# The second expert layer works in expert order, and half of its rows are fetched and transposed while the first layer ends

## The reference

```python
def _moe_ref(x, ...):                      # first layer: one expert for each token
    e_idx = np.argmax(logits, axis=1)
    for e in range(E):                     # E = 8, F = 1024
        mask = e_idx == e
        h = np.maximum(x[mask] @ w1[e], 0.0)
        out[mask] = gate_w[mask, None] * (h @ w2[e])

def _moe2_ref(x, w_gate, w1, w2):          # second layer: every expert for every token
    P = np.exp(x @ w_gate - max)
    for _ in range(8):                     # rows, then columns are scaled
        P /= P.sum(1, keepdims=True) + 1e-09
        P /= P.sum(0, keepdims=True) + 1e-09
        P *= N / E
    for e in range(E):
        out += P[:, e:e + 1] * (np.maximum(x @ w1[e], 0.0) @ w2[e])
```

## Time and profile before

| | us |
|---|---|
| median of 3 runs | 1403.03 (1402.81 to 1403.81) |
| profiled execution, its own time | 1405.03 |
| its span | 1403.0 |
| mean granted TensorE clock | 0.994 |
| TensorE busy | 1371.9 (98%) |
| VectorE / ScalarE / GpSimd busy | 705.2 / 450.6 / 416.4 |

### The profile page before, as it was taken

How to read it: one execution, slowest core, us unless ns; L and a number is a source line. 1 busy time by engine, 2 the same in 40 slices (tenths; PEclk the granted TensorE clock), 3 DMA queues, 4 the chain that set the end, 5 groups by cost and what they waited for, 6 DMA issues and landing times.

```text
span 1403.0 us, 21674 instructions
## 1 busy us (share of the span) xinstructions
PE 1371.9 (98%) x7515; PEld 1221.7 (87%) x7516; DVE 705.2 (50%) x1290; ACT 450.6 (32%) x867; POOL 416.4 (30%) x615
## 2 busy tenths in 40 slices
PE   8999989999799999999999999999999999999999
PEld 7999678888688888999988889999888999988888
DVE  8886672141464644445454444455444445544444
ACT  6887432232243422223131222313122222322221
POOL 4111022222430523415052332505143241605330
PEclk9999999999999999999999999999999999999999
DMA  6440372121301011101110010011101011110001
GB/s 131 107 105 32 129 245 72 42 75 38 136 31 31 30 30 31 31 31 30 45 45 30 30 30 30 30 45 45 30 30 30 30 30 37 43 39 30 30 32 58
DMA packets 95647, 73.85 MB, mean 53 GB/s; under 512 B 43344, under 2 KB 76144, under 8 KB 95600
## 3 DMA queue, kind: packets, MB, share of 16 engines
q1 hardware_dynamic: 92560, 65.34, 15.5%
q0 software_dynamic: 2672, 7.88, 1.7%
q10 hardware_dynamic: 368, 0.02, 0.0%
HBM read 62.74 MB, written 10.49 MB: 52 GB/s over the span
## 4 chain that ended last, share of the span: by engine, by line
PE 92%; DVE 4%; ACT 1%; issue 1%; POOL 1%; DMA 1%; POOLq 0%; SPq 0%; DVEq 0%; ACTq 0%
PE ps L2025 37%; PE ps L2000 33%; PE ps L1886 5%; PE ps L1864 5%; PE ps L1684 3%; PE ps L1618 1%; PE ps L1644 1%; PE ps L1873 1%; PE ps L1630 1%; PE ps L1678 1%; PE ps L1798 1%; PE ps L1603 1%; PE ps L1693 1%; PE ps L1933 1%; PE ps L1844 0%
## 5 line engine op out<-in xcount | busy, mean ns | idle before, releaser
L2000 PE MATMUL ps<-x_hi,w_hi 128*128 128x384 f32 x896 | 301.7, 337 | 4.7 <-DVE x_lo L1447 3.8
L1529 DVE SCALAR_TENSOR_TENSOR acc<-ps,mix,acc 128x512 f32<-128x512 f32 x180 | 135.1, 751 | 329.2 <-PE ps L2025 329.2
L2000 PE MATMUL ps<-x_hi,w_lo 128*128 128x384 f32 x896 | 300.5, 335 | 0.0
L2000 PE MATMUL ps<-x_lo,w_hi 128*128 128x384 f32 x896 | 300.3, 335 | 0.0
L2025 PE MATMUL ps<-w_hi,h_hi 128*128 128x512 f32 x768 | 300.0, 391 | 0.0
L2025 PE MATMUL ps<-w_hi,h_lo 128*128 128x512 f32 x768 | 299.7, 390 | 0.0
L2025 PE MATMUL ps<-w_lo,h_hi 128*128 128x512 f32 x768 | 299.4, 390 | 0.0
L739 POOL TENSOR_TENSOR w_lo<-w_raw,w_hi 128x256 fp32r<-128x256 f32 x224 | 159.0, 745 | 89.5 <-ACT w_hi L934 89.5
L2000 PEld LDWEIGHTS ps<-x_hi,w_hi 128*128 128x128 f32 x896 | 168.9, 188 | 7.6 <-DVE x_lo L1447 4.2
L2025 PEld LDWEIGHTS ps<-w_hi,h_hi 128*128 128x128 f32 x768 | 144.1, 188 | 32.9 <-DVE h_lo L1489 5.0
L2025 PEld LDWEIGHTS ps<-w_hi,h_lo 128*128 128x128 f32 x768 | 144.1, 188 | 30.6
(11 more groups left out here) (280 smaller groups left out, 1781.4 us busy)
## 6 DMA issues: line engine op xcount, KB each, us to landing
w_raw<-in_moe_w_dram SPq DMA_DIRECT2D x64, 256.0 KB, 3.0
w_raw<-in_moe_w_dram SPq DMA_DIRECT2D x16, 1024.0 KB, 5.3
stage<-in_moe_w_dram SPq DMA_DIRECT2D x8, 1024.0 KB, 6.4
first_raw<-in_moe_w_dram SPq DMA_DIRECT2D x4, 1024.0 KB, 8.1
q_raw<-in_q_dram SPq DMA_DIRECT2D x12, 256.0 KB, 3.4
k_raw<-in_k_dram SPq DMA_DIRECT2D x12, 256.0 KB, 4.3
v_all<-in_v_dram SPq DMA_DIRECT2D x12, 256.0 KB, 4.4
x_rows_dram<-x_rows SPq DMA_DIRECT2D x12, 256.0 KB, 4.0
```

What stands on the lines that cost most here:

```text
L1529: dve.scalar_tensor_tensor(out=acc[:, m, :], in0=ps[:, 4 + t % 3, :], scalar=mix_flat[:, bass.ds(e + m * (E + 1), 1)], in1=acc[:, m, :], o ...
L2000: last = pe.matmul(ps[:, bank, 0:CT], w_part[:, j, w, ks], x_part[:, x, k, cols], start=(opens and k == 0 and n == 0), stop=(k == 1 and n ...
```

## The change

**Order.** Results of the first layer stay in order by expert. Instead of scattering a block to its tokens, GpSimd writes it as 128 contiguous rows, starting at `row[b]` (`store_y`); where a block isn't full, the next store covers its tail, since stores are in order. VectorE works out the table `row` before the first layer's loop (7 small operations). The second layer then takes the rows in this order; at the very end the output tiles go to their tokens' rows by a scatter from GpSimd instead of a plain store from SyncE. The token numbers in expert order come from `token_places` (8 small VectorE operations), 12 scatters of 4 bytes per partition to DRAM on GpSimd behind `split_half(0, 1)`, and 12 small loads on SyncE at the end of expert 6.

**Early half.** As soon as the blocks that hold rows 0 to 767 are stored (here 8 of 14), SyncE loads these 6 tiles. They are combined between the last two rests of the first layer, and their seven operands are transposed one operand at a time (6 transposes for an operand): two before the last product's wait, one just before that product, one after it, three between the first products of `up(0, 0, 0)`. The pairs are now (i, i+3) and (i+6, i+9). The first w1 sums and rests move in front of the last stores on GpSimd. w2 is loaded when the last product2 is done, and its first rounding moves to `up(0, 0, 1)`, because w2_hi and w2_lo share memory with the early rows.

```diff
 # SyncE
             load_w1(0, 0)
             load_w1(0, 1)
+            half_done = sp.value_load(tab[0:1, TAB_H:TAB_H + 1], ...)     # blocks - 3
+            half_done = sp.snap(half_done >> 1, ...)
+            for c in range(2):
+                sp.wait_ge(y_buffer_free[c], half_done * 16)
+            for i in range(3):
+                for m in (i, i + 3):
+                    sp.dma_start(y_early[:, m, :], yd[:, m, :]).then_inc(y_loaded[i], 16)
...
+            sp.wait_ge(block_done, last_pair * 2 + 2)
+            load_w2(0, 0)
             sp.wait_ge(y_stored, 1)
-            for i in range(TILES // 2):
-                for m in (i, i + TILES // 2):
-                    sp.dma_start(y_rows[:, m, :], yd[:, m, :]).then_inc(y_loaded[m], 16)
-            load_w2(0, 0)
+            for i in range(3):
+                for m in (i + 6, i + 9):
+                    sp.dma_start(acc[:, m, :], yd[:, m, :]).then_inc(y_loaded[i + 3], 16)
 # GpSimd
-            for c in range(2):
-                scatter_y(last_pair, c, last_pair * 4 + (c + 2))
...
+            sums_w1(0, 0)
+            sums_w1(0, 1)
+            lows_w1(0, 0)
+            store_y(last_pair, 0)
+            lows_w1(0, 1)
+            store_y(last_pair, 1)
...
             hold(6).then_inc(y_stored, 1)
-            split_half(0, 0)
+            split_w2(0, 0)
...
             split_half(0, 1)
+            pool.wait_ge(places_ready, 1)
+            for m in range(TILES):
+                pool.indirect_dma_start(out=tokens_dram, out_offset=...token_place[:, m:m + 1]...,
+                                        in_=token_id[:, m:m + 1], ...).then_inc(tokens_placed, 16)
...
+                    pool.wait_ge(out_bank_free, 24 * (E - 1) + u * 6 + t + 1)
+                    pool.indirect_dma_start(out=out, out_offset=...row_token[:, m:m + 1]..., in_=acc[:, m, :], ...)
 # ScalarE
+            act.wait_ge(xr_loaded[0], last_pair * 16 + 32)
+            act.wait_ge(xr_loaded[1], last_pair * 16 + 16)
             w1_round(0, 0)
-            for i in range(3):
-                x2_round(i)
+            hT_round(last_pair, 1)
             w1_round(0, 1)
-            up_evacuate(0, 0, 0)
+            act.wait_ge(block_done, last_pair * 2 + 2)
+            for n in range(4):
+                early_round(n)
+            up_evacuate(0, 0, 0, after_p1=next_early, hook=lambda: early_round(6))
...
-                w2_now = u % 2 == 0 and j == 0
+                w2_now = u % 2 == 0 and j == (1 if begin and u == 0 else 0)
 # VectorE
+            hT_rest(last_pair, 0)
+            split_next(last_pair, 0)
             for i in range(3):
                 x2_combine(i)
-            for i in range(3):
-                x2_rest(i)
+            token_places()
+            y_evacuate(last_pair, 0)
+            hT_rest(last_pair, 1)
+            y_evacuate(last_pair, 1)
+            for n in range(4):
+                early_rest(n)
+            up_finish(0, 0, 0, after_u2=lambda: early_rest(4), after_u3=lambda: early_rest(5),
+                      after_c11=lambda: early_rest(6))
             x2_combine(3)
-            up_finish(0, 0, 0)
+            dve.wait_ge(y_stored, 1)
             up_finish(0, 0, 1)
 # TensorE
             transpose_h(last_pair * 2 + 2)
-            keep_busy(14, 0)
-            product2(1, last_pair * 2 + 1, last_pair * 2 + 2)
-            keep_busy(90, 0)
-            for i in range(3):
-                transpose_y(i)
-            up(0, 0, 0)
+            pe.wait_ge(x2_combined, 3)
+            transpose_early(0)
+            transpose_early(1)
+            keep_busy(4, 5)
+            pe.wait_ge(hT_split, last_pair * 2 + 2)
+            transpose_early(2)
+            product2(1, last_pair * 2 + 1, last_pair * 2 + 2)
+            pe.wait_ge(y_copied, last_pair * 2 + 2)
+            transpose_early(3)
+            up(0, 0, 0, behind={"P1": transpose_early_4, "P7": transpose_early_5, "P2": transpose_early_6})
```

More of the change, by code:

```diff
@@ L127, in attention_moe_moe @@
         idx_x = take("idx_x", [PART, 2], i32)
-        idx_y = take("idx_y", [PART, 2], i32)
+        token_id = take("token_id", [PART, TILES], i32)
+        place_f = take("place_f", [PART, TILES])
+        token_place = take("token_place", [PART, TILES], i32)
+        row_token = take("row_token", [PART, TILES], i32)
+        row_f = take("row_f", [PART, 24])
+        row = take("row", [PART, 24], i32)
         used = take("used", [PART, 1])
@@ L330, in attention_moe_moe @@
         table_ready = sem("table_ready")
+        rows_ready = sem("rows_ready")
+        places_ready = sem("places_ready")
+        tokens_placed = sem("tokens_placed")
+        row_tokens_loaded = sem("row_tokens_loaded")
         shifted = sem("shifted")
@@ L421, in tile_of @@
         def tile_of(u, t):
-            return (t // 3) * (TILES // 2) + (u % 2) * 3 + t % 3
+            return (u % 2) * (TILES // 2) + t
         def head_of(half, l):
@@ L749, in split_half, with store_y @@
             def split_half(e, hu):
-                split_w1(e, 2 * hu)
-                split_w1(e, 2 * hu + 1)
+                for p in (2 * hu, 2 * hu + 1):
+                    sums_w1(e, p)
+                    lows_w1(e, p)
                 split_w2(e, hu)
-            split_half(0, 0)
+            def store_y(i, c):
+                pool.wait_ge(y_copied, i * 2 + (c + 1))
+                pool.wait_ge(y_buffer_free[1 - c], i * 16 + (16 + 16 * c))
+                at_row = pool.value_load(row[0:1, bass.ds(i * 2 + c, 1)], min_val=0, max_val=N)
+                pool.dma_start(y_rows_dram[bass.ds(at_row, PART), :], y_blk[:, c, :]).then_inc(y_buffer_free[c], 16)
+            pool.wait_ge(rows_ready, 1)
+            with pool.Fori(0, PAIRS - 1) as i:
+                with pool.If(i < last_pair):
+                    for c in range(2):
+                        pool.wait_ge(xT_done, i * 2 + (c + 2))
+                        gather_x(i * 2 + (c + 3), 1 - c, i * 2 + (c + 2))
+                        store_y(i, c)
+            sums_w1(0, 0)
[4 more added lines that the diff above has]
+            store_y(last_pair, 1)
+            pool.wait_ge(y_buffer_free[0], pairs * 16 + 16)
+            pool.wait_ge(y_buffer_free[1], pairs * 16 + 16)
+            hold(6).then_inc(y_stored, 1)
+            split_w2(0, 0)
             pool.wait_ge(local_max, 1)
@@ L1975, in up @@
                 cols = slice((u % 2) * CT, (u % 2 + 1) * CT)
-                if begin and u < 2 and j == 0:
-                    pe.wait_ge(x2_split, 3 * u + 3)
+                if begin and u == 1 and j == 0:
+                    pe.wait_ge(x2_split, OPS + 3)
                 if u % 2 == 0:
                     pe.wait_ge(w1_split, e * 4 + (2 * (u // 2) + j + 1))
-                for name, bank, w, x in PRODUCTS:
+                for n, (name, bank, w, x) in enumerate(PRODUCTS):
+                    if first:
+                        pe.wait_ge(x2_split, n + 1)
                     if name == "P1" and not first:
@@ L1998, in up @@
                         ks = slice(k * PART, (k + 1) * PART)
-                        for n, (w_part, x_part) in enumerate(((w1_hi, x2_hi), (w1_hi, x2_lo), (w1_lo, x2_hi))):
+                        for h, (w_part, x_part) in enumerate(((w1_hi, x2_hi), (w1_hi, x2_lo), (w1_lo, x2_hi))):
                             last = pe.matmul(ps[:, bank, 0:CT], w_part[:, j, w, ks], x_part[:, x, k, cols],
-                                             start=(opens and k == 0 and n == 0), stop=(k == 1 and n == 2),
+                                             start=(opens and k == 0 and h == 0), stop=(k == 1 and h == 2),
                                              skip_group_check=True)
@@ L2031, in down @@
                             step()
-            for i in range(3):
-                transpose_y(i)
-            up(0, 0, 0)
+            transpose_h(last_pair * 2 + 1)
+            product1(1, last_pair * 2 + 1, last_pair * 2 + 2)
+            product2(0, last_pair * 2, last_pair * 2 + 1)
+            transpose_h(last_pair * 2 + 2)
+            pe.wait_ge(x2_combined, 3)
[8 more added lines that the diff above has]
+            up(0, 0, 0, behind={"P1": transpose_early_4, "P7": transpose_early_5, "P2": transpose_early_6})
             up(0, 0, 1)
```

254 lines of the change are left out of this document (147 added, 107 removed).

## The result

The changed kernel takes 1397.19 us, median of 7 runs (1395.80 to 1399.25), against 1403.03 us for the kernel before in the same job (7 runs, 1402.79 to 1404.72). The ratio is 0.9959, 95% interval 0.9947 to 0.9970: 5.8 us faster. Forecast were 1389.6 us, with a range of 1384 to 1397: the median lies 0.2 us above the range. The direction was right; less than half of the gain of 13.4 us came.

A forecast was written before the change was run, and what follows sets the result against it. TensorE, busy 98% of the span, was taken as the bound; down(0, 0) 16.7 us earlier, less 2.1 for one clock fall, with 1.2 added for the last store, gave -13.4 from 1403.03: 1389.6 us, range 1384 to 1397.

The forecast's parts named there:

- the last store: Kernel's end: a GpSimd scatter instead of a plain store adds 1.2 us (0.8 to 4.8).
- sign of a span end: Sign of being right: span ends 3.2 us or so after the last accumulation.
- Product2: First layer's last product: ends 3.1 us later than 360.83; its start 2 to 4 us after 355.09 was a sign.
- The combining: Twelve VectorE operations before the last product: 9.8 us beside GpSimd's work, bounds 5.0 and 11.4 us.
- The w2 wait: Before down(0, 0): TensorE waits about 3.2 us for GpSimd's w2 rests, bounds 2 and 5 us.
- the first up product: Start of the second layer: P1 starts at 365.9; 364 to 368 was named as a sign of being right.
- the window of 13 to 18: Sign of being right: down(0, 0) starts 13 to 18 us before 403.76; forecast 16.7 us earlier at full clock.
- The clock: Two new TensorE holes, 2.7 and 3.2 us; one fall of the granted clock counted, costing 2.1 us.
- Rival B: Both holes cost clock and VectorE is disturbed throughout (combining 11.4 us, token_places doubled): 1394 us, chance 22%.
- The rest of the change: Row table, plain loop stores, early loads, and token scatters and loads: each counted as 0 us.
- C: Early chain ends only behind the last store because VectorE meets it late: 1403 us, no change, chance 5%.
- D: Token scatters hold GpSimd at 6.4 us each, second expert's weights 39 us late: 1429 us, chance 6%.

The follow-up runs named there:

- b1: Kernel before the change, with GpSimd doing one tiny operation behind the last accumulation; 1405.84 us, ratio 1.0006.
- e8: Changed kernel with two tiny operations behind the last scatter's completion, one on VectorE and one on GpSimd; 1398.83 us, ratio 0.9959.
- e9: Changed kernel, but GpSimd starts its first weight sums only after VectorE combined the three early pairs; 1392.70 us, ratio 0.9910.
- c2: Changed kernel with SyncE doing the last wait, token_places behind the last rest, earlier w2 rounding, GpSimd's sums behind the combining; 1387.00 us, ratio 0.9875.
- e10: Changed kernel with the twelve last tiles as plain sync-queue stores, GpSimd doing one tiny operation behind the last accumulation; 1394.98 us, ratio 0.9936.
- e3: Changed kernel, but SyncE instead of GpSimd waits for the twelve scatters at the end; 1394.97 us, ratio 0.9930.
- e4: Changed kernel, but GpSimd issues twelve plain stores instead of twelve scatters at the end and still waits for them; 1397.42 us, ratio 0.9950.
- b3: Like b2, but the 24 added DMAs are one instruction in a loop of 24 rounds; 1408.19 us, ratio 1.0027.
- b2: b1 plus 24 more 32-byte DMAs that GpSimd issues and waits for before the last accumulation ends; 1407.07 us, ratio 1.0018.
- e7: Changed kernel with twenty idle TensorE transposes between up(0, 0, 1) and down(0, 0)'s wait on the w2 rests; 1395.77 us, ratio 0.9940.
- e5: Changed kernel, but VectorE computes token_places behind the rest of the last hidden block; 1392.95 us, ratio 0.9914.

## Why the prediction was wrong, and where it was right

**The failing step is the last store**: "about 0.4 us to get going, 2.8 to land. +1.2 us (0.8 to 4.8)". It was sized at 1.2 us and measured 6.25. The two sizes in it were right (0.27 us to the scatter's start, 2.7 to 2.8 from there to completion); what comes after GpSimd's last instruction it left as it was. GpSimd ended before at 1347.91 us, so its own way to the end was hidden under 55 us (not under some 20, as b1's expectation has it). Now that GpSimd finishes last, that way stands in the open: 3.5 us with 39 DMAs issued, and about 0.08 us more for each of the next 24. With 63 DMAs that is 5.5 us. Of the 2.4 us before, 2.0 were the plain store itself, and 0.4 was left. The profile of before could not have given the number, since nothing in it ended last on GpSimd; but the bounds were drawn from how long a scatter takes, and what else depends on the engine that ends last wasn't asked. With 6.25 in place of 1.2 the same sum gives 1394.7, inside the range. The far bound of 4.8 us did not reach it either. The forecast's sign of a span end "3.2 us or so" behind the last accumulation is not its own sum, which gives 2.4 + 1.2 = 3.6. The Trainium skill, DMA: Bandwidth & Descriptors, Specifications, on which the prediction's estimate of +0.4 us rests, speaks of first bytes alone, and the end of the program is no part of it. Up to completion the traces have 2.7 to 2.8 us for the scatter (e8) against 2.0 for the plain store, a difference of 0.7 to 0.8 us where the estimate has 0.4.

**Product2 was 2.1 us later than forecast, beyond the 1.7 us that block 11 was late.** It started at 361.95, and without those 1.7 us 5.2 later than the 355.09 of before, where 3.1 was forecast and 2 to 4 was named as a sign of being right. 1.10 us is a stretch of issue ahead of the first combining operation that the sum didn't have. The combining took 10.1 us (forecast 9.8) and the small operations 3.1 (2.4): their first two, 0.75 and 0.65 us, still ran beside GpSimd. That is 2.1. The mechanism was right (each combining took 0.83 to 0.96 us, the first apart), and e9 shows its worth: 4.4 us of the 5.2 by which the stage grew. The Trainium skill, SBUF — State Buffer, "SBUF: two separate sides", says that the loser of the shared port waits for the winner's whole instruction. The traces agree in size: in c2 a rest of 0.55 us and a combining of 0.42 take 1.64 and 1.50 beside GpSimd operations of 1.5, while in the changed kernel GpSimd operations of 0.73 to 0.93 make 0.42 into 0.83 to 0.96.

**The w2 wait** was forecast at 3.2 and came at 2.74; the first up product came at 369.67 less 1.67, 2.1 late as product2 was; up(0, 0, 0) stalled for 0.36 us (forecast 0.5) and up(0, 0, 1) for 0.28 (forecast 0.75). Down(0, 0) was early by 13.4 us, at the lower end of the window of 13 to 18.

**The clock**: one fall at full price was counted, 2.1 us; at down(0, 0) it cost 1.83. There were two. In the profiled execution the other one, at 356 to 360 us, came while TensorE was waiting for VectorE's list anyway, and was over before the product: no cost of it can be seen. In seven of the ten profiles above it lies inside the last product and costs 1.6 us more (27.8 us from block 11 to block 13 instead of 26.2). So the forecast's one fall is too few for most executions; of the 2.5 us between 1394.7 and the median this and the late product2 are the likely parts. Rival B had both falls; its other half, combining at 11.4 us, did not come.

**The rest of the change** was rightly counted at nothing in the places that the forecast looked at. The token scatters take 1.0 us each with 0.3 between, from 468.8 to 484.0, and GpSimd waits 17.24 us for w1 behind them, against 32.39 before:

```profile
483.02 0.96 POOL L786 DMA_INDIRECT tokens_dram<-token_id,token_place  x1 [0.30 <-issue]
501.21 0.73 POOL L721 TENSOR_TENSOR w_raw<-w_raw 128x256 f32<-128x256 f32 x1 [17.24 <-DMA w_raw<-in_moe_w_dram]
```

Rivals C and D are out. But these twelve scatters are not free after all: by e10's count they stand for 1.0 us of the longer end.

The 1.7 us by which block 11 was late are not the change's: e3 and e4 have the same code up to there and evacuate block 11 at 337.70, and b1 and b3, which have the code of before, at 337.81 and 337.59. All four are without the falls at 20 to 30 and at 190 us. So the table of rows costs nothing there, as forecast.

## What to carry to other kernels

Ask of a change which engine will end last. An engine that was done long before the end may carry a cost on its way out that no profile shows until it is last; a tiny operation put behind the last completion on each engine finds it in one run. Keep GpSimd from the end, or let another engine do the last wait; and count its DMAs. Where GpSimd is given work earlier, look at what VectorE does at the same time: here a start behind the combining gave back 4.4 of 5.2 us and added no wait.

## What was unexpected of the hardware

- From the end of GpSimd's last instruction to the end of the span: 3.5 us with 39 DMAs issued by it, 4.5 with 51, 5.45 to 5.8 with 63, also where they had completed tens of microseconds before (b2, b3). What it does in that time, and why it grows so, no run shows.
- Plain store or scatter by indices on GpSimd makes no difference to it (e4: 8.0 us from issue to the end, the changed kernel 8.4, of which 0.4 is the longer issue).
- The clock's falls at 20 to 30 and at 190 us come in some executions of the same code and not in others, and block 11 moves between 337.6 and 342.4 us with them. What decides it stays open.
- One fall of the clock behind TensorE's idle 2.7 us costs 1.8 us (down(0, 0) to the last accumulation, 997.92 against 996.09 without it), and twenty idle transposes in the hole keep it away (e7). In e5's profile, where the clock stays low from 384 to 391 us, it costs 3.0.
